# Attention scores held in twenty-two places instead of six, and another sequence on each engine

## The reference

```python
scores = scale * np.matmul(q, k.transpose(0, 1, 3, 2))
kth = np.partition(scores, -top_k, axis=-1)[..., -top_k:-top_k + 1]
mask = scores >= kth
scores = np.where(mask, scores, -1000000000.0)
attn = np.exp(scores - np.max(scores, axis=-1, keepdims=True))
attn = attn / (np.sum(attn, axis=-1, keepdims=True) + 1e-09)
x = tokens_by_channels(np.matmul(attn, v))            # 2304 x 512
x = (1.0 / (1.0 + np.exp(-(x @ w_gate))) * (x @ w_val)) @ w_out       # 512 -> 1536 -> 512
r = np.maximum(x @ w_in, 0.0)                         # 512 -> 2048
return (r * r) @ w_out2                               # 2048 -> 512
```

## Time and profile before

| | us |
|---|---|
| median of 3 runs | 1213.51 (1213.34 to 1213.71) |
| the profiled execution | 1213.16 |
| its span, first to last instruction | 1211.3 |
| outside the span | 1.86 |

### The profile page before, as it was taken

One profiled execution on the slowest core, in us unless ns is written; L12 is line 12 of the kernel. 1 busy time (PEld: TensorE's weight loads), 2 busy tenths in 40 slices (PEclk: granted clock), 3 DMA queues, 4 the chain that ended last, 5 costly groups with the idle time before them and its releaser, 6 DMA issues.

```text
span 1211.3 us, 21823 instructions
## 1 busy us (share of the span) xinstructions
PE 1159.8 (96%) x7520; PEld 1001.7 (83%) x7520; DVE 845.9 (70%) x1756; ACT 740.9 (61%) x1758; POOL 626.7 (52%) x539
## 2 busy tenths in 40 slices
PE   4679999999989999999999999999999999999999
PEld 2458888998889999988877777777878788899998
DVE  7989989697698789899687769994667576001130
ACT  6887778777686776777665647765555466112130
POOL 5876577766676554566454535653444266012030
PEclk9679999999999999999999999999999999999999
DMA  9978776998769776666655455556454445577784
GB/s 360 339 256 258 253 257 216 324 291 268 253 225 314 226 221 203 227 200 214 224 177 171 157 190 195 179 188 206 154 183 164 167 157 175 173 256 249 260 245 146
DMA packets 90397, 270.13 MB, mean 223 GB/s; under 512 B 10032, under 2 KB 16176, under 8 KB 90288
## 3 DMA queue, kind: packets, MB, share of 16 engines
q1 hardware_dynamic: 90288, 268.74, 66.6%
HBM read 228.33 MB, written 40.37 MB: 222 GB/s over the span
## 4 chain that ended last, share of the span: by engine, by line
PE 81%; ACT 7%; DVE 5%; POOL 4%; issue 2%; DMA 1%; SPq 0%; ACTq 0%; POOLq 0%; DVEq 0%
PE ps L583 20%; PE ps L585 19%; PE ps L584 19%; PE ps L524 7%; PE ps L569 6%; PE ps L485 6%; PE ps L501 5%; POOL below L833 2%; DVE top L767 2%; DVE work L769 2%; ACT below L620 1%; ACT scores L615 1%; DVE g_lo L804 1%; ACT probs L634 1%; ACT below L627 1%
## 5 line engine op out<-in xcount | busy, mean ns | idle before, releaser
L833 POOL TENSOR_TENSOR below<-scores,below 128x576 f32<-128x576 f32 x144 | 205.8, 1429 | 266.8 <-ACT below L627 263.9
L767 DVE MAX8 top<-work 128x8 f32<-128x576 f32 x432 | 312.1, 750 | 5.0
L583 PE MATMUL ps<-xy_hi,ring 128*128 128x512 f32 (+2 forms) x800 | 290.0, 362 | 2.0 <-ACT act_buf L693 2.0
L585 PE MATMUL ps<-xy_hi,ring 128*128 128x512 f32 (+2 forms) x800 | 282.0, 352 | 0.0
L584 PE MATMUL ps<-xy_lo,ring 128*128 128x512 f32 (+2 forms) x800 | 281.6, 352 | 0.0
L769 DVE MATCH_REPLACE8 work<-top,work 128x576 f32<-128x576 f32 x288 | 213.8, 742 | 0.0
L583 PE MATMUL ps<-g_hi,ring 128*128 128x384 f32 (+2 forms) x560 | 201.8, 360 | 0.5 <-POOL g_lo L862 0.5
L585 PE MATMUL ps<-g_hi,ring 128*128 128x384 f32 (+2 forms) x560 | 197.1, 352 | 0.0
L584 PE MATMUL ps<-g_lo,ring 128*128 128x384 f32 (+2 forms) x560 | 196.7, 351 | 0.0
L838 POOL TENSOR_TENSOR probs<-probs,rinv 128x576 f32<-128x576 f32 x128 | 149.7, 1169 | 41.9 <-DVE rinv L782 41.9
L583 PEld LDWEIGHTS ps<-xy_hi,ring 128*128 128x128 f32 x800 | 150.6, 188 | 21.5 <-issue 6.2
(11 more groups left out here) (58 smaller groups left out, 1758.0 us busy)
## 6 DMA issues: line engine op xcount, KB each, us to landing
ring<-w_split SPq DMA_DIRECT2D x318, 512.0 KB, 3.8
wring<-w_in SPq DMA_DIRECT2D x113, 256.0 KB, 4.8
w_split<-stage SPq DMA_DIRECT2D x46, 512.0 KB, 5.0
w_split<-ring SPq DMA_DIRECT2D x22, 512.0 KB, 6.2
vt<-v_in SPq DMA_DIRECT2D x16, 480.0 KB, 5.2
heads_in<-qk_in SPq DMA_DIRECT2D x16, 336.0 KB, 4.4
vt<-v_in SPq DMA_DIRECT2D x16, 320.0 KB, 3.4
heads_in<-qk_in SPq DMA_DIRECT2D x16, 304.0 KB, 4.1
```

Of the source, the lines that this page charges most:

```text
L583: nc.tensor.matmul(dst, w_hi, hi[:, k, 0:WIDTH[c]], start=first, stop=False)
L585: mm = nc.tensor.matmul(dst, w_lo, hi[:, k, 0:WIDTH[c]], start=False, stop=final)
L767: nc.vector.max(out=best, in_=sc if step == 0 else wk).then_inc(sel_step[t % 2], 1)
L833: nc.gpsimd.tensor_tensor(out=below[:, t % 2, :], in0=scores[:, t % PLACES, :], in1=below[:, t % 2, :], op=ALU.subtract).then_inc(mask_don ...
```

## The change

`SCORE`, `PLACES` and the fixed rule for score slots give way to a planner with 11 places of its own and 11 more ("spare") laid over buffers that only the split MLPs use. Until the first MLP starts (slot 15) it scores one unit in every slot in which places are free; afterwards a unit is scored three slots ahead of its first tile, as before. Worked out from the planner, units 0 to 3 are scored in slots -3, -1, 0 and 1, then one unit in each slot up to unit 16 in slot 14; the next, unit 17, comes in slot 24, and from there every unit has the slot that it had before. Before, unit 3 was scored in slot 2, unit 4 in slot 3, unit 8 in slot 9 and unit 11 in slot 14, and units 12 to 16 in slots 16, 18, 19, 21 and 23. The loads of q and k move with the scores (groups 3 to 7 from slots 3, 6, 9, 14 and 19 to slots 2, 4, 6, 9 and 12). The number of half blocks of chunk 0 in each slot follows from the planner of `shares`, which spreads PE's work evenly.

```diff
-AHEAD = 5
-STORE_LAG = 3
+AHEAD = 4
+STORE_LAG = 2
...
-PLACES = 6
-
-SCORE = 3
-SCORE_AT = {FIRST_OF[u] - SCORE: u for u in range(NU)}
+SCORE, PLACES, SPARE = 3, 11, 11
+
+
+def score_plan():
+    at, place, prev = {}, [], []
+    free_at = {i: (0, None) for i in range(PLACES + SPARE)}
+
+    def put(u, s):
+        for t in (t for t in range(NT) if TILES[t][0] == u):
+            stay = s >= MLP_AT[0]
+            i = min((i for i in free_at if i < PLACES or not stay), key=lambda i: (max(free_at[i][0], s), i < PLACES, i))
+            place.append(i)
+            prev.append(free_at[i][1])
+            free_at[i] = (t + MASK, t)
+        at[s] = u
+
+    u = 0
+    for s in range(-SCORE, NT):
+        if u == NU:
+            break
+        free = sum(free_at[i][0] < s for i in free_at if i < PLACES or s < MLP_AT[0])
+        must = FIRST_OF[u] - SCORE <= s
+        if must or s < MLP_AT[0] and free >= (1 if UNITS[u][4] else 2):
+            put(u, s)
+            u += 1
+    return at, place, prev
...
-    HEADS_AT.setdefault(max(FIRST_TILE[_g - 1] - 3, 0), []).append(_g)
+    HEADS_AT.setdefault(max(SCORE_SLOT[FIRST_UNIT[_g - 1]], 0), []).append(_g)
...
-    SPLIT_AT.setdefault(_k * (MLP_AT[0] - 1) // NPRE, []).append(_k)
+    SPLIT_AT.setdefault(1 + _k * (MLP_AT[0] - 2) // NPRE, []).append(_k)
...
             def copy_scores(t):
-                wait(act, mask_done, t - PLACES + 1)
+                if PLACE_OF_AHEAD[t] is not None:
+                    act.wait_ge(mask_done, PLACE_OF_AHEAD[t] + 1)
...
                 if c >= NW and 2 <= n <= 2 * NJ1 and n % 2 == 0:
                     j = n // 2 - 1
+                    if c == NW and j == 0:
+
+                        wait(act, mask_done, LAST_SPARE + 1)
...
                     find_below(s - MASK)
                     enlarge(s - MASK)
-
+                for k in SPLIT_AT.get(s, []):
+                    split_weights(k)
                 if s - 1 in PROD_AT:
                     copy_x(PROD_AT[s - 1])
...
                 if last:
                     copy_pt(PROD_AT[s])
+                if last:
+                    copy_x(PROD_AT[s])
                 if 0 <= s - MASK:
                     exp(s - MASK)
                 if s in PROD_AT and not last:
                     copy_pt(PROD_AT[s])
-                for k in SPLIT_AT.get(s, []):
-                    split_weights(k)
-                if last:
-                    copy_x(PROD_AT[s])
             for s in range(MLP_AT[0], SLOTS):
...
+                if s in PROD_AT:
+                    copy_pt(PROD_AT[s])
                 for c, n in blocks_of(SHARES[s - 1][2]):
                     evac(c, n)
-                if s in PROD_AT:
-                    copy_pt(PROD_AT[s])
                 for c, p in X_AT.get(s, []):
                     split_x(c, p)
+                for c, n in blocks_of(SHARES[s][0]):
+                    evac(c, n)
                 if s - MASK < NT:
                     exp(s - MASK)
-                for c, n in blocks_of(SHARES[s][0]):
-                    evac(c, n)
...
             for s in range(SLOTS):
-                select_both(s, [0, 1])
+                select_both(s, [0])
                 if s in NORM_AT and s >= MLP_AT[0]:
                     invert(NORM_AT[s])
+                select_both(s, [1])
                 for c, n in blocks_of(SHARES[s - 1][2]) if s else []:
                     evac(c, n)
                 select_both(s, [2])
+                for c, n in blocks_of(SHARES[s][0]):
+                    evac(c, n)
+                select_both(s, [3])
+                for c, n in blocks_of(SHARES[s][1]):
+                    evac(c, n)
                 if s in NORM_AT and s < MLP_AT[0]:
                     invert(NORM_AT[s])
-                for c, n in blocks_of(SHARES[s][0] + SHARES[s][1]):
-                    evac(c, n)
-                select_both(s, [3])
...
+                for c, n in blocks_of(SHARES[s - 1][2]) if s else []:
+                    evac(c, n)
                 for k in SPLIT_AT.get(s - 1, []):
                     split_weights(k)
-                for c, n in blocks_of(SHARES[s - 1][2]) if s else []:
-                    evac(c, n)
```

More of the change, by code:

```diff
@@ L155 @@
 PROD_SLOT = {u: s for s, u in PROD_AT.items()}
-PLACES = 6
-SCORE = 3
 FIRST_OF = [min(t for t in range(NT) if TILES[t][0] == u) for u in range(NU)]
-SCORE_AT = {FIRST_OF[u] - SCORE: u for u in range(NU)}
+SCORE, PLACES, SPARE = 3, 11, 11
[20 more added lines that the diff above has]
+    return at, place, prev
+SCORE_AT, PLACE_OF, PLACE_OF_AHEAD = score_plan()
+SCORE_SLOT = {u: s for s, u in SCORE_AT.items()}
+LAST_SPARE = max([t for t in range(NT) if PLACE_OF[t] >= PLACES], default=-1)
 SLOTS = MLP_AT[NC - 1] + 1
@@ L251, in attention_mlps @@
         with nc.sbuf_tensor("y0", [P, NM, NMAX], F32) as y0, nc.sbuf_tensor("x0", [P, NM, NMAX], F32) as x0, \
-                nc.sbuf_tensor("g0", [P, NJ2, NMAX], F32) as g0:
+                nc.sbuf_tensor("g0", [P, NJ2, WIDTH[0]], F32) as g0, \
+                nc.sbuf_tensor("spare_hi", [P, 8, SEQ], F32) as spare_hi:
             pass
@@ L257, in attention_mlps @@
         with nc.sbuf_tensor("stage", [P, STAGES, 2, KT * P], F32R) as stage, \
-                nc.sbuf_tensor("x1", [P, NM, NMAX], F32) as x1:
+                nc.sbuf_tensor("spare_lo", [P, 3, SEQ], F32) as spare_lo:
             pass
@@ L275, in x_of, with scores_of @@
         def x_of(c):
-            return (x0, x1)[c] if c < NW else xf
+            return x0 if c < NW else xf
+        def scores_of(t):
+            i = PLACE_OF[t]
+            return scores[:, i, :] if i < PLACES else spare_hi[:, i - PLACES, :] if i < PLACES + 8 else spare_lo[:, i - PLACES - 8, :]
         def early(u):
@@ L469, in score @@
                 wait(pe, s_copied, FIRST_OF[u])
-                ahead = sum(TURN_SLOT[v] < FIRST_OF[u] - SCORE for v in range(NU))
+                ahead = sum(TURN_SLOT[v] < SCORE_SLOT[u] for v in range(NU))
                 if part == 1 and ahead and not early(ahead - 1):
@@ L494, in turn @@
                     wait(pe, s_copied, max([t + 1 for t in range(NT) if TILES[t][1] == 1
-                                            and FIRST_OF[TILES[t][0]] - SCORE <= TURN_SLOT[u]], default=0))
+                                            and SCORE_SLOT[TILES[t][0]] <= TURN_SLOT[u]], default=0))
                     wait(pe, x_done, u)
@@ L601, in _ @@
                     times_v(PROD_AT[s])
-                for c, h in SHARES[s][1] + SHARES[s][2]:
+                for c, h in SHARES[s][1]:
+                    mlp_half(c, h)
+                for c, h in SHARES[s][2]:
                     mlp_half(c, h)
@@ L611, in copy_scores @@
             def copy_scores(t):
-                wait(act, mask_done, t - PLACES + 1)
+                if PLACE_OF_AHEAD[t] is not None:
+                    act.wait_ge(mask_done, PLACE_OF_AHEAD[t] + 1)
                 act.wait_ge(s_scored, t + 1)
                 bank = score_bank(t)
-                nc.scalar.activation(two(scores[:, t % PLACES, :]), ps[:, bank:bank + 2, 0:HALF], ACT.Copy).then_inc(s_copied, 1)
+                nc.scalar.activation(two(scores_of(t)), ps[:, bank:bank + 2, 0:HALF], ACT.Copy).then_inc(s_copied, 1)
             def find_below(t):
                 act.wait_ge(sel_step[t % 2], 7 * (t // 2 + 1))
-                nc.scalar.activation(below[:, t % 2, :], scores[:, t % PLACES, :], ACT.Sign,
+                nc.scalar.activation(below[:, t % 2, :], scores_of(t), ACT.Sign,
                                      bias=top[:, t % 4, TOPK - 1:TOPK], scale=-1.0).then_inc(sign_done, 1)
@@ L757, in select @@
             def select(t, step):
-                sc, wk, tp = scores[:, t % PLACES, :], work[:, t % 2, :], top[:, t % 4, :]
+                sc, wk, tp = scores_of(t), work[:, t % 2, :], top[:, t % 4, :]
                 if step == 0:
@@ L832, in mask @@
                 pool.wait_ge(below_done, t + 1)
-                nc.gpsimd.tensor_tensor(out=below[:, t % 2, :], in0=scores[:, t % PLACES, :], in1=below[:, t % 2, :],
+                nc.gpsimd.tensor_tensor(out=below[:, t % 2, :], in0=scores_of(t), in1=below[:, t % 2, :],
                                         op=ALU.subtract).then_inc(mask_done, 1)
```

## The result

The kernel before took 1213.61 us (median of 4 runs, 1213.34 to 1215.07), the changed one 1197.43 us (4 runs, 1197.10 to 1199.10): a ratio of 0.9869, 95% interval 0.9853 to 0.9884. So 16.2 us came off, where 13 were forecast, and the time lies inside the range, though nearer to the 1198 of the first rival (the fast early stretch) than to the forecast 1200.5. The profiled execution took 1197.49 us, its span is 1195.7.

A forecast was written before the change was run, and what follows sets the result against it. TensorE was taken as the bound from 83.38 us, VectorE's select ahead of it. Terms -4.9 - 0.4 - 3.5 - 5.5 - 0.8 + 1.0 + 1.0 = -13.1 took 1213.16 to 1200.1; forecast 1200.5 us (chance 0.48), range 1195.5 to 1209.

The forecast's parts named there:

- the first rival: Ahead of the first MLP: extra scores bring TensorE's full clock, first block at 81.4 to 82.3, whole 1198 us; chance 0.14.
- 4.9 + 0.4: First MLP: 4.9 us off for scores of units 12 to 16 moved earlier, 0.4 for a turn's wait going with them.
- early +1.0: Ahead of the first MLP: first block at 84.4 us instead of 83.38, so 1.0 us longer.
- 5.5, with 0.8 for the clock: Beside the MLPs: copy_pt earlier takes 5.5 us off scores' waits for copied transposes; 0.8 more from the low clock behind.
- 3.5: Beside the MLPs: exp behind share 0's evacuation removes 3.5 us of stalls from tanh and relu queued behind mask waits.
- the wait at its third block: First MLP: the 1.53 us stall at 89.07 us; its absence was a sign of being right.
- 1.0 for new gaps: Beside the MLPs: 1.0 us set aside for new gaps from the later evacuation and exp; bounds 0 and 25.
- the longest stall: Second MLP, at 335.96 us: a score waited 2.41 us; clock 0.58 and 0.57 behind it, cost 1.7 us, 0.8 counted.
- 83 to 86 us: Start of the first MLP block: the range that would show the forecast right; after 88 us would show it wrong.
- The walk through slots 3 to 14: Ahead of the first MLP: step-by-step timing at the low clock gave the first block at 85.7 us, with faster pieces 82.3.
- works where it waited: Beside the MLPs: VectorE does step 3 between two shares instead of behind both; no price, since TensorE is the bound.
- 5 us for 2 us of work: Beside the MLPs: AHEAD 4 gives a split four blocks, 5 us and more, for 2 us of work; priced at nothing.

The follow-up runs named there:

- trace at 0.53: The kernel after with AHEAD 5 and STORE_LAG 3 as before; three runs gave 1202.38, 1203.76 and 1200.06 us, ratio 0.9906.
- orders-only kernel: The kernel after with its scores put back in their old slots and six places, all new orders kept: 1201.67 us, ratio 0.9902.
- doubled scores: The kernel before with every score matmul of units scored ahead of the first MLP issued twice: 1217.17 us, ratio 1.0029.

## Why the prediction was right, and where it wasn't

| edit undone in the kernel after | costs by the medians, us | by the ratios, us | term forecast |
|---|---|---|---|
| score plan | 4.2 | 4.0 | 4.9 + 0.4, less part of the early +1.0 |
| copy_pt ahead of the evacuation | 6.5 | 5.6 | 5.5, with 0.8 for the clock |
| exp behind the evacuation | 3.8 | 2.2 | 3.5 |
| ScalarE's early order | 3.3 | 3.3 | none of its own |
| VectorE's order | 2.3 | 2.4 | 0 |
| AHEAD and STORE_LAG | 3 to 6 | 4.5 | 0 |

Each ratio has an interval of about 0.0015, or 1.8 us, to either side, so the costs of 2.2 and 2.4 us are at the edge of what can be told.

**Right.** The moved scores: TensorE's busy time in the first MLP fell by 4.96 us for a forecast 4.9. The first MLP lasts 128.63 us (127 to 128 forecast, so 0.6 over), the wait at its third block is gone, and scores wait 2.7 us for copies (under 3). The part behind the third MLP hasn't moved.

**Right in sum, in part by luck: the three MLPs.** They and the rest are 13.9 us shorter where the terms without the early one made 14.1. But TensorE's idle time there fell by 5.8 us, where the terms for waits (0.4 + 3.5 + 5.5 less 1.0 for new gaps) made 8.4. The waits for copied transposes fell by 4.6 for 5.5, and turns wait 1.3 us for copied scores where it was 1.2, so the forecast 0.4 did not come. Busy time fell by 8.2 us, where 4.9 + 0.8 was forecast: the clock behind the longest stall was put at 0.8, and 3.2 us of busy time are gone from the second and third MLP, whose clock is 1.00 now. The two misses cancel. That the clock holds in the kernel after is not settled by the edits either: behind the wait for g_lo it fell in three kernels that differ from this one by a single edit. The prediction called it full wherever TensorE has no gaps; its own have TensorE without a gap at 0.58 and 0.57.

**Mis-sized: the early stretch.** The term was +1.0 and measured -1.68, and with it the miss of 3 us is nearly all accounted for (-13.1 forecast, -15.6 in the spans). The first block at 81.70 us misses the 83 to 86 named as a sign of being right. The walk through slots 3 to 14 took the low clock's lengths and made ScalarE the bound at 14.8 of 15.25 us. It had ScalarE's slot 9 start at 52.3 us, pushed back by the weight split now ahead of it; it started at 51.18, since the splits run in the 11.2 us in which ScalarE used to wait for masks. The walk then waits 1.0 us for unit 4's product, where 0.25 was measured, and its pieces of TensorE are too long (products of 1.89 and 1.31 us for 2.40, a half unit's turn 0.77 for 1.33). At the low clock itself it would still have been too long: in the trace at 0.53 the first block started at 83.57, not 85.7. That 85.60 came in the kernel with the plan and the old orders is coincidence, as the walk was made for the new ones. The orders' share is the 3.1 us between 84.81 and 81.70. What the plan costs here isn't shown: the four kernels with one and the same program up to slot 14 (the one after, those with exp or copy_pt put back, and that with copy_pt further ahead) start the first block at 81.70, 81.75, 81.95 and 80.71, and the orders-only kernel's 80.74 lies in that spread. VectorE's pace set the time: it is busy 21.66 of the 22 us from 45 to 67, as the row shows, though the clock is only 0.74:

```profile
45.00:67.00 22.00, 14.87 (x119) 9.78 (x115) 21.66 (x49) 20.93 (x52) 20.01 (x17) 0.74 0.92 322
```

The first rival had this outcome (81.4 to 82.3) with another cause, the full clock. The time it gave for the stretch was right and its reason wrong.

**New gaps.** 1.0 us was set aside; 1.8 us for g_lo is what came, in one place, behind VectorE's select, beside 0.5 us in two short waits for a 0.5 us that is gone.

**Costed at nothing and wrong: VectorE's order, and AHEAD with STORE_LAG.** Both were argued from cover on average: VectorE "works where it waited", and a split has 5 us for 2 us of work. Undone, they cost 2.3 and about 5 us. The cover has holes, as the 338.49 row of POOL shows for a split in front of an evacuation; that AHEAD's share comes from this is an argument, not shown. POOL's own new order (evacuation ahead of the split) was not tried alone.

**The terms aren't independent.** The six costs add up to 25 us by the medians and 22 by the ratios, the whole change gave 16.2. From the other side, the plan alone and the early order alone give 1.0 and 0.7 us by their ratios, both within their intervals of nothing. Part of this is the clock behind a stall: of the 25 us, 2.0 and 2.4 are busy time at a low clock in the profiled executions without exp's and without copy_pt's new place, and 1.7 of the 3.1 us that the early order won alone went the same way. The rest is a reading, not shown by itself: TensorE is held by one in-order ScalarE queue with several stalls close together, and with one taken away the next grows and keeps what was won, as the stall of 1.53 us that became 2.76. The same edit is then worth nothing first and 3 or 4 us last.

## What to carry to other kernels

On an engine that works in order, an instruction costs its own time plus every wait of what stands ahead of it: look through the evacuation to the operand it waits for, on whatever engine, before pricing a move. Put work that is ready into the gap ahead of one that waits for another engine, and be wary of one that waits for the bottleneck ahead of what the bottleneck's next input is made from; here that last step was the way from 1197 to 1219 us. Edits that loosen one queue have to be measured together as well as singly, since each alone can show nothing. And before a difference between two kernels is put down to an edit, compare TensorE's busy time as well as its waits: the clock behind a stall can hold in one trace and fall in the next.

## What the runs showed of the hardware

VectorE's select took 22.48 us for four tiles with TensorE's granted clock at 0.50 and 22.52 us with 0.85: a faster TensorE doesn't shorten a stretch that VectorE ends.

The length of a wait alone doesn't decide whether the granted clock falls behind it. Six traces have the wait of 1.8 to 1.9 us for g_lo in the second MLP. In three (after, ScalarE's old early order, early load of group 2) the clock stayed at 1.00; in the other three (orders only, exp put back, VectorE's order put back) it stood at 0.50, the lower of its two levels (1.2 of 2.4 GHz), for two of the microseconds behind the wait, and TensorE's busy time in that MLP was 1.6 to 2.0 us longer. Behind the wait of 2.4 us for copied transposes it fell in the kernel before and in that with the early order alone, and stayed at 1.00 in the plan-alone kernel and in that with doubled scores. What decides it isn't shown by these runs.
